# Second mixture in two fp16 pieces instead of two fp32r pieces, with scales found at run time

## The reference

```
# 1: delta rule: 4 batches x 8 heads x 768 steps, state 48x48
y[t]  = q[t] @ state
state = state + beta[t] * outer(kn[t], v[t] - kn[t] @ state)
x = y as (3072 tokens, 384)
# 2: first mixture: 8 experts, each token goes to at most one
h = relu(x[mask] @ w1[e]);  x[mask] += gate * (h @ w2[e])       # w1: 384x1024, w2: 1024x384
# 3: second mixture: dense, all 3072 tokens
h = relu(x @ w_in);  out = (h * h) @ w_out                      # w_in: 384x2048, w_out: 2048x384
```

## Time and profile before

| | us |
|---|---|
| median of 3 runs | 974.9 (974.88 to 984.97) |
| the profiled execution's own time | 973.0 |
| its span, first to last instruction | 971.0 |
| PE busy | 911.8 (94%) |
| DVE busy | 498.4 (51%) |
| ACT busy | 444.8 (46%) |
| POOL busy | 310.3 (32%) |

### The profile page before, as it was taken

How to read it: one execution, slowest core, us unless ns; L and a number is a source line. 1 busy time by engine, 2 the same in 40 slices (tenths; PEclk the granted TensorE clock), 3 DMA queues, 4 the chain that set the end, 5 groups by cost and what they waited for, 6 DMA issues and landing times.

```text
span 971.0 us, 27385 instructions
## 1 busy us (share of the span) xinstructions
PE 911.8 (94%) x11591; PEld 826.6 (85%) x11592; DVE 498.4 (51%) x994; ACT 444.8 (46%) x803; POOL 310.3 (32%) x305
## 2 busy tenths in 40 slices
PE   8999999999999982999999399999999999999998
PEld 4888888888888871999999289899999899898897
DVE  5666767777676653445545543333333333343332
ACT  5666666675666660455454333333333333332322
POOL 6456567666667653255454200000000000000000
PEclk9999999999999995899999599999999999999999
DMA  7333433644342211265655500010100200100200
GB/s 209 114 114 99 129 107 101 194 126 126 115 117 78 81 41 36 93 216 170 245 210 199 196 1 1 8 58 1 55 12 1 65 0 0 65 0 0 65 1 32
DMA packets 39223, 84.45 MB, mean 87 GB/s; under 512 B 9656, under 2 KB 29786, under 8 KB 36816
## 3 DMA queue, kind: packets, MB, share of 16 engines
q1 hardware_dynamic: 36176, 77.89, 25.3%
q0 software_dynamic: 2944, 5.05, 1.6%
HBM read 67.16 MB, written 17.42 MB: 87 GB/s over the span
## 4 chain that ended last, share of the span: by engine, by line
PE 82%; DVE 7%; DMA 5%; issue 2%; ACT 2%; POOL 1%; DVEq 0%; SPq 0%; POOLq 0%; ACTq 0%
PE h L1492 21%; PE acc L1508 21%; PE h L1416 5%; PE bX L806 4%; PE bX L823 3%; PE acc L1428 3%; DMA raw<-wts 3%; PE bU L827 3%; PE yb L896 3%; PE mb L880 3%; PE yb L889 3%; PE kb L917 3%; PE gB L846 2%; PE gA L846 2%; DVE X L657 2%
## 5 line engine op out<-in xcount | busy, mean ns | idle before, releaser
L1379 DVE SCALAR_TENSOR_TENSOR sqr<-h,relu 128x512 f32<-128x512 f32 x96 | 66.5, 692 | 186.9 <-ACT relu L1266 186.9
L1266 ACT ACTIVATE relu<-h 128x512 f32<-128x512 f32 x96 | 57.4, 598 | 195.0 <-PE h L1492 194.8
L1508 PE MATMUL acc<-w_hi,hl 128*128 128x384 f32 x384 | 129.8, 338 | 0.0
L1508 PE MATMUL acc<-w_hi,hh 128*128 128x384 f32 x384 | 129.6, 338 | 0.0
L1508 PE MATMUL acc<-w_lo,hh 128*128 128x384 f32 x384 | 129.1, 336 | 0.0
L657 DVE TENSOR_TENSOR X<-bX,cst 128x512 f16<-128x512 f32 x120 | 82.7, 689 | 89.3 <-PE bX L806 89.3
L1492 PE MATMUL h<-xh,w_hi 128*128 128x512 f32 x288 | 115.9, 402 | 1.4 <-DVE xl L1361 1.4
L1492 PE MATMUL h<-xh,w_lo 128*128 128x512 f32 x288 | 114.8, 398 | 0.0
L1492 PE MATMUL h<-xl,w_hi 128*128 128x512 f32 x288 | 114.6, 398 | 0.0
L1382 DVE TENSOR_TENSOR hl<-sqr,hh 128x512 fp32r<-128x512 f32 x96 | 66.5, 693 | 67.1 <-ACT hh L1268 67.1
L1268 ACT ACTIVATE hh<-sqr 128x512 fp32r<-128x512 f32 x96 | 60.7, 633 | 73.2 <-DVE sqr L1379 73.2
(11 more groups left out here) (161 smaller groups left out, 1938.4 us busy)
## 6 DMA issues: line engine op xcount, KB each, us to landing
raw<-wts SPq DMA_DIRECT2D x18, 1536.0 KB, 7.1
kq<-kqT SPq DMA_DIRECT2D x24, 448.0 KB, 4.0
R<-kv SPq DMA_DIRECT2D x24, 384.0 KB, 4.2
x_rows<-xs SPq DMA_DIRECT2D x48, 192.0 KB, 4.2
rows_in<-x_rows SPq DMA_DIRECT2D x8, 768.0 KB, 4.7
kn<-k_rows SPq DMA_DIRECT2D x24, 192.0 KB, 2.7
out<-rows_out SPq DMA_DIRECT2D x24, 192.0 KB, 1.9
raw_w<-first_w SPq DMA_DIRECT2D x24, 128.0 KB, 3.4
```

Of the source, the lines that this page charges most:

```text
L1266: act.activation(relu[:, f % 2], hb[f % 2][:], ACT.Relu).then_inc(m_relu, 1)
L1379: dve.scalar_tensor_tensor(out=sqr[:, f % 2], in0=hb[f % 2][:], scalar=0.0, in1=relu[:, f % 2], op0=ALU.max, op1=ALU.mult).then_inc(m_sqr, 1)
L1508: last = pe.matmul(acc[sub][:, 0:DM], h[:, f % 4, sub * P:(sub + 1) * P], w[1][:, f // 8].rearrange("p (f d) -> p f d", f=8)[:, f % 8], st ...
```

## The change

The second mixture's operands become fp16: high part and low part are both fp16, and the three products stay. Since fp16 has a small range, everything is scaled by powers of two first and scaled back at the end:

- Weights: the largest absolute value of `w_in` and of `w_out` is needed. Before their turn to be split, in steps 0 to 5 of stage 2, SP loads a third of a unit a step (128x2048 fp32, 1 MB, `scan_w`), three steps' worth for each of the two units, and DVE takes the largest absolute value (`scan`, a tensor_reduce and a small maximum). The load is SP's first instruction of the step, behind the previous step's reload of half 1. `scan` stands on DVE behind `split_lo` of half 0 chunk 2, ahead of `hidden_lo` 2. In step 6 SP writes the 128x2 maxima to DRAM, waits, and reads them back broadcast to all partitions; DVE waits for that where `scan` stood, and makes the scales (`weight_scales`). ACT's copy of a weight chunk then multiplies by the scale (`scaled_hi`) and DVE's subtraction too (`scaled_lo`, a scalar_tensor_tensor).
- Rows: for each tile DVE sums the absolute values of each row (128x1536 in one tensor_reduce) and makes scales (`row_scales`, six instructions); ACT multiplies the rows in place, four instructions of 128x384 (`scale_rows`); the transposes wait for that, and move to f = 8, 10, 12.
- The relu takes an immediate scale, and both drains multiply by a scale for each row (`row_down`).
- In step 7, and for unit 9, POOL splits nothing: DVE makes all three chunks of half 0. Unit 9's half 1 is split within the first tile, at f = 1, 2, 3, and `m_layer2` waits for it at f = 8 alone.
- The loop over pairs of experts runs three times, and the last two steps are written out.

The diff, cut to its core:

```
+SCAN = HALF * 2 * P // 3 // P
@@ SP, in step(e)
+                if not isinstance(e, int):
+                    sp.dma_start(scan_w[:], second_w[par][bass.ds(P * j, P)]).then_inc(scan_in, 16)
+                elif e == E - 2:
+                    sp.wait_ge(w_max_set, E - 1)
+                    sp.dma_start(w_max_dram, w_max[:]).then_inc(w_max_out, 16)
+                    sp.wait_ge(w_max_out, 16)
+                    sp.dma_start(w_max_all[:], w_max_dram.rearrange("(o p) u -> o (p u)", o=1).broadcast_to([P, 2 * P]))\
+                        .then_inc(w_max_in, 16)
                 for half in range(2):
                     sp.wait_ge(w_lo_ready[half], 3 * (e + 1))
                     load(e + 2, half)
@@ POOL, in step(e)
-                for c in range(2):
-                    split_lo(e + 1, 1 - par, c)
+                if not last(e):
+                    for c in range(2):
+                        split_lo(e + 1, 1 - par, c)
@@ ACT
+            def scaled_hi(u, half, par, chunk):
...
+                act.activation(w_hi_half[par][:, half, cols], raw[:, half, cols], ACT.Copy,
+                               scale=w_up[:, u - E:u - E + 1]).then_inc(w_hi_ready[half], 1)
...
+            def scale_rows(t, par):
+
+                act.wait_ge(row_up_ready, t + 1)
+                for a in range(B):
+                    rows = rows_in[:, par, DM * a:DM * (a + 1)]
+                    act.activation(rows, rows, ACT.Copy, scale=row_up[:, par, a:a + 1]).then_inc(rows_scaled, 1)
@@ DVE
+            def scan(e, par):
+
+                dve.wait_ge(scan_in, 16 * (e + 1))
+                dve.tensor_reduce(chunk_max[:, par:par + 1], scan_w[:], AX_X, ALU.max, apply_absolute_value=True).then_inc(scanned, 1)
+                dve.wait_ge(scanned, e + 1)
+                dve.tensor_tensor(w_max[:, par:par + 1], w_max[:, par:par + 1], chunk_max[:, par:par + 1], ALU.max)\
+                    .then_inc(w_max_set, 1)
...
             def step(e, par, j):
                 hidden_lo(first, e, 0)
                 hidden_lo(first, e, 1)
-                split_lo(e + 1, 1 - par, 0, 2)
+                split = scaled_lo if last(e) else split_lo
+                if last(e):
+                    for c in range(2):
+                        split(e + 1, 1 - par, 0, c)
+                split(e + 1, 1 - par, 0, 2)
+                if not isinstance(e, int):
+                    scan(e, par)
+                elif e == E - 2:
+                    weight_scales()
                 hidden_lo(first, e, 2)
                 hidden_lo(first, e, 3)
...
+            def row_scales(t, par, loads):
+
+                dve.wait_ge(x2_in[par], 16 * loads)
+                dve.tensor_reduce(row_norm[:], rows_in[:, par, 0:4 * DM].rearrange("p (a d) -> p a d", a=B), AX_X, ALU.add,
+                                  apply_absolute_value=True).then_inc(row_steps, 1)
...
@@ PE
-                        w, x = (w_hi, w_lo)[b], (xh, xl)[a]
+                        w, x = (w_hi_half, w_lo_half)[b], (xh_half, xl_half)[a]
...
-                        h, w = (hh, hl)[a], (w_hi, w_lo)[b]
+                        h, w = (hh_half, hl_half)[a], (w_hi_half, w_lo_half)[b]
```

More of the change, by code:

```diff
@@ L1059, in blocks, with last @@
         def blocks(eng, step):
-            with eng.Fori(0, E // 2) as j:
+            with eng.Fori(0, E // 2 - 1) as j:
                 step(2 * j, 0, j)
                 step(2 * j + 1, 1, j)
+            step(E - 2, 0, E // 2 - 1)
+            step(E - 1, 1, E // 2 - 1)
+        def last(e):
+            return isinstance(e, int) and e == E - 1
         def further(eng, e, body):
@@ L1070, in further @@
                     body(j, b + j)
+        second_w = [wts[E + u].rearrange("h p c -> (h p c)").rearrange("(r c) -> r c", c=SCAN) for u in range(2)]
         def w1_of(w, par):
@@ L1259, in drain @@
                         act.wait_ge(stored, 64 * t)
-                    act.activation(rows_out[:, a], acc[a][:, 0:DM], ACT.Copy).then_inc(m_drained[0], 1)
+                    act.activation(rows_out[:, a], acc[a][:, 0:DM], ACT.Copy, scale=row_down[:, par, a:a + 1])\
+                        .then_inc(m_drained[0], 1)
             def tile(t, par, j):
@@ L1265, in tile @@
                     act.wait_ge(m_h_full, n + 1)
-                    act.activation(relu[:, f % 2], hb[f % 2][:], ACT.Relu).then_inc(m_relu, 1)
+                    act.activation(relu[:, f % 2], hb[f % 2][:], ACT.Relu, scale=SQUARE_SHIFT).then_inc(m_relu, 1)
                     act.wait_ge(m_sqr, n + 1)
-                    act.activation(hh[:, f % 4], sqr[:, f % 2], ACT.Copy).then_inc(m_hi, 1)
+                    act.activation(hh_half[:, f % 4], sqr[:, f % 2], ACT.Copy).then_inc(m_hi, 1)
                     if f == 1 and not (isinstance(t, int) and t == 0):
-                        drain(t - 1)
-                    if f in (5, 7, 9) and not (isinstance(t, int) and t == NC - 1):
-                        t_hi(t + 1, (f - 5) // 2, 1 - par)
+                        drain(t - 1, 1 - par)
+                    if f in (1, 2, 3) and isinstance(t, int) and t == 0:
+                        scaled_hi(E + 1, 1, 1, f - 1)
+                    if f == 5 and not (isinstance(t, int) and t == NC - 1):
+                        scale_rows(t + 1, 1 - par)
+                    if f in (8, 10, 12) and not (isinstance(t, int) and t == NC - 1):
+                        t_hi(t + 1, (f - 8) // 2, 1 - par)
             tiles(act, tile)
-            drain(NC - 1)
+            drain(NC - 1, 1)
         @block.vector
@@ L1475, in m_transposes @@
                 if kd == 0:
-                    pe.wait_ge(x2_in[par], 16 * loads)
+                    pe.wait_ge(rows_scaled, B * (t + 1))
                 for i in range(4):
@@ L1497, in m_layer2 @@
                 n = 16 * t + f
-                if isinstance(t, int) and t == 0 and f == 0:
-                    for half in range(2):
-                        pe.wait_ge(w_lo_ready[half], 3 * (E + 1))
+                if isinstance(t, int) and t == 0 and f % 8 == 0:
+                    pe.wait_ge(w_lo_ready[f // 8], 3 * (E + 1))
                 if f == 0 and not (isinstance(t, int) and t == 0):
```

162 lines of the change are left out of this document (118 added, 44 removed).

## The result

The changed kernel takes 971.6 us (median of 20 runs, 965.8 to 982.1), the kernel before 974.8 in the same series (20 runs, 971.8 to 985.0). The ratio is 0.995, 95% interval 0.992 to 0.997; it leaves out the slowest executions, and the rest come in two groups some 9 us apart, whatever the kernel, as stage 1 ends at 388 to 392 us in some profiled executions and at 397 to 399 us in others (there the clock is at 1.2 GHz for 17.1 us from about 30 us on). The forecast was 958 us with a range of 949 to 970, so the time is above the range: a gain of 17 us was expected, and some 5 are there by the ratio.

The account below looks back on a forecast made before the run. PE was taken to bound stage 3 by its pitch, and a loop of loads and splits stage 2. -28.6 + 3.9 + 6.8 + 0.2 + 0.5 + 0.5 = -16.7 us on 973.0; forecast 958 us, range 949 to 970.

Parts of the forecast that it names:

- PE's pitch: Stage 3: fp16 matmuls at 0.2167 and 0.1635 us make a piece 3.91 us instead of 4.21, 28.6 us less.
- five drains: Stage 3: PE waits 0.1 us a tile for the accumulators' drains, +0.5 us for five tiles (0 to 1.5).
- Rival (c): Stage 3: fp16 products of real data keep 0.233 and 0.176 us, only costs are left, 987 us; chance 0.05.
- The way into stage 3: Between landed rows and transposes: DVE's sum, two small instructions and ACT's four copies, all bare, +3.9 us (3.5 to 4.6).
- Moving it gains nothing: Ahead of stage 3: splitting unit 9's half 1 later saves 0 us, as the wait for rows covered it.
- The search: Stage 2, steps 1 to 5: the scan's load and reduction make a step 19.35 us against 18.0, +6.8 us.
- rival (b): Stage 2: POOL's pair shuts out the reduction, 3.4 us a step, 17 for five, 968 us; chance 0.13.
- rival (d): Stage 2: PE stalls above 3.5 us drop its clock, some 2 us more each, past 975 us; chance 0.04.
- Rival (a): Stage 2: the scan is hidden, DVE starting it before hl(2) is due; 6.8 us goes, 951 us; chance 0.17.
- Step 6: Stage 2: the 1 KB of maxima written out and read back makes 18.6 us against 18.0, +0.5 us (0 to 3).
- Step 7: End of stage 2: two extra low parts on DVE (2.4 us) lie in its idle time and cost nothing.
- step 0: Start of stage 2: load issued long before, so only the 2.3 us reduction counts, against PE's later need: +0.2 us.

Follow-up runs that it names:

- lo_after_scatter: Changed kernel, but DVE waits for the last scatter to land before unit 9's three low parts of half 0; 973.0 us, ratio 0.988 to the kernel before.
- max_one_input: Changed kernel, but the small running maximum is a tensor_reduce over two columns in one buffer; 966.3 us, ratio 0.988 to the kernel before.
- load_ahead: Changed kernel, but the scan's load is issued a step earlier, the two-input maximum staying; 973.5 us, ratio 0.997 to the kernel before.
- no_search: Changed kernel without the search's loads, reductions and 1 KB round trip, weight scales being constants; 959.3 us, ratio 0.978 to the kernel before.
- ahead_one_late: load_ahead plus max_one_input, with `weight_scales` behind DVE's low parts in step 6; 961.7 us, ratio 0.985 to the kernel before.
- all_moved: ahead_one_late plus lo_after_scatter, last reload behind the first tile's rows, DVE scaling two of four row blocks; 961.8 us, ratio 0.982 to the kernel before.

## Why the prediction was wrong

**PE's pitch: right.** 0.2156 and 0.1625 us against 0.2167 and 0.1635 forecast from stage 1's rows. The pieces give 29.5 us, less 0.8 behind five drains (forecast -28.6 and +0.5). That the sum came out within 0.6 us is in part luck: a piece gave 0.31 us for 0.298, and the first 27 products, over half of their time at the lower clock, gave nothing where I had counted all 96 pieces. Rival (c), that the type doesn't set the pitch, fell.

**The way into stage 3: right in kind, 0.9 too small.** +4.8 for +3.9. Landed rows to transposes was 4.47 us where I had 3.8; the four copies with a scale operand took 2.13 us, not 1.63. The other 0.3 us lie ahead of that: the first work on the landed rows began 12.5 us after the last output's end instead of 12.2. The scatters' doubled issues are not the cause of any loss that a run shows: without them, in lo_after_scatter, the stretch was 22.1 us. "Moving it gains nothing" held.

**The search: the step that failed.** I had +6.8 for steps 1 to 5; it was +15.2. The wait for the load, the term that I had, was about the right size: max_one_input, which has it without the lock, comes to +7.4 once its two falls are taken off. What I had put at nothing makes the rest: by 1.5 us a fall, some 4.5 us are the three falls of the clock and some 3.3 the lock (estimates). Two sentences of that step are wrong. The first is "with the small maximum 0.2 more that the next one doesn't wait for". That instruction has two inputs in SBUF, and I had the row that shows what POOL does to such a one, and the row that POOL's pair runs just there. I put both to the 2.3 us reduction, as rival (b), and not to the 0.2 us maximum behind it; DVE works in order, so hl(2) waits for it whether it reads it or not. The reduction itself was never shut out: (b) as I put it fell, its mechanism came by the neighbour. The Trainium skill, "SBUF — State Buffer", section "Who interferes with whom", has both halves: two SBUF inputs contend with GpSimd's reads, a tensor_reduce doesn't. By that rule the traces agree: up to 3.63 us for the 128x1 tensor_tensor (load_ahead), and 2.29 for the reduction inside the pair against 2.27 in step 0, where no pair runs. It also names tensor_scalar among those that can take the shared ports, and the 5.30 us in no_search agree.

The second is in rival (d): "my stalls are near 1.4 us, at most 2.7, and none should let it fall". I had read a threshold of 3.5 us from one idle stretch. In this kernel the clock fell in steps whose stalls were 2.92, 3.00 and 1.77 us and didn't in those of 1.74, 1.85 and, in step 6, 3.15. The same steps in lo_after_scatter had stalls of 2.98 and 3.00 us without a fall and one of 1.84 with one. So the stall's length alone doesn't decide, and no threshold can be read from these rows. A fall cost 1.4 to 1.6 us, for which I had "some 2" without a row; how many of them a given execution has is chance as far as these runs show.

Rival (a), that the scan is hidden, fell with PE's stalls. The loads were not the matter as such: in step 2 the scan's data landed 0.8 us earlier than I had reckoned, and with the load a step ahead and the one-input maximum, steps 1 to 5 cost 1.5 us in all. What I forecast, DVE waiting for the load, was there (12.4 us in five steps) but hid behind the lock and the lock behind it: taking away the wait gave 2.1 us of 15.2, taking away the lock 4.8, taking both 13.7.

**Step 6: +3.2 for +0.5.** hl(2) ended 15.1 us after the reload's issue (513.74), where I had 13.2: SP came to the 1 KB store only 2.2 us after the reload, and it landed 10.7 us after it, for 8.25 forecast. PE stood for 3.15 us, and SP's later wait didn't make that good. Moving `weight_scales` took 5.0 us from step 6 in the experiment, some 2.5 of them a long fall of the clock.

**Step 7, costed at nothing: +0.8.** Here I named the low parts and not the written-out code. PE's stop of 1.27 us is a wait for instructions that are still being loaded, and it goes when PE runs a loop.

**Sum.** -29.5 + 0.8 + 4.8 + 15.2 + 3.2 + 0.8 - 0.3 (step 0) - 0.3 (stage 1) = -5.3, the measured -5.4.

Open: why the load of instructions for step 7 began ahead of l1(0) in seven kernels and some 2.3 us behind its start in two, where PE then stopped for 3.5 us. (The DMA engines were busy 81% of 520 to 524 us in ahead_one_late and 27% of 533 to 536.3 after, but no run changes that alone.) Why the clock fell behind one stall of 1.77 us and not behind 3.15 is open as well. Open too is whether moving the reload would be enough without DVE's wait, as all_moved changed them together; the wait without the move gave nothing.

## What to carry to other kernels

Where an engine works in order, price each added instruction, the smallest too, by what it can be held by: here a maximum of two columns, 0.16 us when alone, held DVE for 0.8 to 3.6 us behind a 2.3 us reduction that nothing held up. Two causes that end at the same moment hide each other, so a cost that is removed alone shows only the difference to the next; test them in pairs. A stall of PE cost another 1.4 to 1.6 us in clock in some steps, even one of 1.8 us, so near a full PE ask for no stall rather than for a short one. And before a difference between two single profiles is put down to an edit, look at a pair with the same work: here it was up to 3 us in five steps.

## What the runs showed of the hardware

- DVE instructions of one or two columns were held to the end of POOL's whole pair of instructions: a tensor_tensor up to 3.63 us, a tensor_scalar 5.30 us, where the two POOL instructions together took 4.72; a tensor_reduce was never held (2.28 us beside the pair, 2.27 without).
- POOL's indirect scatters took 1.9 and 2.1 us to issue beside DVE's scalar_tensor_tensor with two SBUF inputs, 1.0 us without.
- At the first execution of new code, PE's next product came 1.25 to 1.5 us after a 16 KB transfer of instructions had ended. Depending on when that transfer began, PE stopped for 0 to 3.5 us.
- Behind a stall of PE the clock fell to 1.2 GHz for 3.4 or 6.8 us in some steps and not in others with the same stall (3.00 us with and without, after and lo_after_scatter).
- The scatter of rows landed 0.5 to 0.9 us behind a 1536 KB reload issued ahead of it (six kernels), whether its own issue had taken 1.0 or 2.1 us.
- A 1 KB store behind a 1536 KB load took 8.5 us to land.
